# The order of work in the first four chunks of a fused attention and two-MLP kernel

## The chip, the cores and the metric

The kernel runs on one core of a Trainium2 chip. What is measured is the device time of one execution in microseconds. The core has five engines that work side by side, each through its own instructions in their written order: TensorE (PE: matmuls), VectorE (DVE), ScalarE (ACT), GpSimd (POOL) and SyncE (SP), which here only issues loads and stores. They meet through semaphores: an instruction raises one when it is done, and an engine stands still at a wait until the value is there.

## The reference, cut to what matters

```python
# attention, 4 x 8 heads, 576 tokens, head_dim 64, window of 64 tokens
scores = scale * q @ k.T;  scores masked with -1e9 outside the window
attn = exp(scores - rowmax) / (rowsum + 1e-9);  x = attn @ v         # 2304 x 512 tokens
# first MLP ("A"), d_ff 1536
xn = x / sqrt(mean(x * x) + 1e-6) * rms_g
x2 = (silu(xn @ w_gate) * (xn @ w_val)) @ w_out
# second MLP ("B"), d_ff 2048
h = x2 @ w_in;  out = (h * sigmoid(1.702 * h)) @ w_out2
```

All is float32. Each factor is split into a high part (rounded to a type that TensorE takes at full rate) and a low part (the rest), and each product is three matmuls: high by high, low by high, high by low (lines 646 to 649).

## The kernel before, in words

MLP A goes over five tiles of tokens, `TILES_A` (line 38): tile 0 has 256 tokens, the others 512. In each tile it goes over `CA` = 12 chunks of 128 columns of d_ff. A chunk c has three matrices of weights m: gate (0), value (1) and output (2), each 128x512, written here as (c, m). They are loaded in tile 0 only and stay in `w_all`.

**A chunk on TensorE** (lines 747 to 768): `gate(t, c)`, `val(t, c)` of 12 matmuls each, and two chunks later `project_A`, again 12. Between them stands the attention of the next tile, in steps of 256 tokens and two heads: steps 4 to 11 in tile 0 (`EARLY` = 4 steps were done before). A pair of steps is in work over three chunks (`SCORES_AT` = 1, 3, 5, 7): scores after chunk 1, row maxima, exponentials and normalisation with chunk 2, transposes with chunk 3 (line 614), the multiplications by V (`probs_by_v`, line 628), then the next pair's scores (line 600). `probs_by_v(4, 3)` waits until hidden of chunk 2 is made (line 621), since its result goes to the PSUM bank that val of chunk 2 was in. `val(0, 4)` in its turn waits until ScalarE has copied that result away (line 698).

**A chunk on VectorE** in tile 0: `scale_gate` (line 1249), `silu_A` (1254, after ScalarE's tanh), `hidden_A` (1263), `hid_lo_A` (1269, after ScalarE's cast `hid_hi_A`). Between them stand the low halves of the weights two chunks ahead, `weights_lo_A` (line 1218), each of which raises `w_split`, and for a pair of steps `row_max` (1133), `reciprocal_of_sum` (1143, 1145) and `normalise` (1150). `row_max` of a pair waits for the scores of both steps.

**A chunk on ScalarE:** `tanh_A` (line 996), `hid_hi_A` (1006), the high halves of the weights three chunks ahead, `weights_hi_by_act` (920), for a pair of steps `exponentials` (881), `copy_probT` (908) and `evacuate_o` (874). The high halves of the third matrix (m = 2) are GpSimd's (546).

**Loads** are issued by SyncE. The raw weights of chunks c and c + 2 share one staging buffer, so `load_wA(c, m)` (line 402) first waits until (c - 2, m) is split. The wait is for a count, so `FIRST_SPLITS` (line 276) has to hold the order in which VectorE makes its splits. In tile 0, iteration c issues the three loads of chunk c + 3, then q and k of the next pair of steps where there is one, then v.

The orders of the four engines are written out by hand in these loops; there is no planner.

Of the kernel before, what the change touches and what calls it, by code (L numbers as in the profile page):

```python
# [23 lines left out]
def fused_attention_mlps(nc, q_t, k_t, v_win, w_a, rms_g, w_b, out):  # L24
# [5 lines left out]
    CA = w_a.shape[0]  # L30
# [20 lines left out]
    EARLY = 4  # L51
# [15 lines left out]
    with ExitStack() as ctx:  # L67
# [205 lines left out]
        def raw(u, m):  # L273
            return wstage[:, (3 * u + m) * DM:(3 * u + m + 1) * DM]

        FIRST_SPLITS = ((0, 0), (0, 1), (1, 0), (1, 1), (2, 0), (0, 2), (2, 1), (1, 2), (2, 2))

        def splitsA(c, m):
            return FIRST_SPLITS.index((c, m)) + 1 if c < 3 else 3 * c + m + 1

        CASTS_BY_ACT = ((0, 1), (1, 1), (2, 0), (2, 1)) + tuple((c, m) for c in range(3, CA) for m in range(2))
        CASTS_BY_POOL = ((0, 0), (1, 0), (0, 2), (1, 2)) + tuple((c, 2) for c in range(2, CA))
# [108 lines left out]
        @block.sync  # L391
        def _(sp):
            def load_step_qk(s):
                sp.wait_ge(scores_done, s - 1 if s >= EARLY + 2 else s - EARLY + 1)
                load_q(sp, s)
                load_k(sp, s)

            def load_step_v(s):
                sp.wait_ge(pv_done, s - 1 if s >= EARLY + 2 else s - EARLY + 1)
                load_v(sp, s)  # L400

            def load_wA(c, m):
                if c >= 2:
                    sp.wait_ge(w_split, splitsA(c - 2, m))
                sp.dma_start(raw(c % 2, m), w_a[c, :, m * DM:(m + 1) * DM]).then_inc(w_loaded[c % 2][m], 16)

            def load_w2(k):
                g, m = (k // 2 - 1, 1) if k % 2 == 0 and k > 0 else ((k + 1) // 2, 0)
                f = 2 * (g % PB)
                if k >= RAWS:  # L410
                    sp.wait_ge(w2_split, pieces_before(k - RAWS + 1))
                sp.dma_start(raw2(k).rearrange("p (f n) -> p f n", f=2),
                             w_b[f:f + 2, :, m * DM:(m + 1) * DM].rearrange("f p n -> p f n")
                             ).then_inc(w2_loaded[k % RAWS], 16)

            def store_x2(t):
                start, n = TILES_A[t]
                for i in range(2):
                    sp.wait_ge(accA_evacuated[i], 2 * (t + 1))
                sp.dma_start(x2[:, :, start:start + n].rearrange("c p t -> p c t"),  # L420
                             x2stage(t)[:, :, 0:n]).then_inc(x2_stored, 16)

            def load_x2(j):
                wait(sp, xcB_lo, COMBOS * j)
                sp.dma_start(x2raw[:, :, :], x2[:, :, j * TB:(j + 1) * TB].rearrange("c p t -> p c t")
                             ).then_inc(x2_loaded, 16)

            def store_out(j):
                for s in range(SUB):
                    sp.wait_ge(accB_evacuated[s % 2], (SUB // 2) * j + s // 2 + 1)  # L430
                    start = j * TB + s * P
                    sp.dma_start(out[start:start + P, :], yB[:, s, :]).then_inc(out_stored, 16)

            for s in range(EARLY):
                load_q(sp, s)
            sp.dma_start(gcol[:, :], rms_g).then_inc(g_loaded, 16)
            for m in range(3):
                load_wA(0, m)
            for m in range(3):
                load_wA(1, m)  # L440
            load_wA(2, 0)
            for s in (EARLY, EARLY + 1):
                load_step_qk(s)
            load_wA(2, 1)
            for s in (EARLY, EARLY + 1):
                load_step_v(s)
            load_wA(2, 2)

            for t in range(NA - 1):
                for c in range(CA):  # L450
                    if t == 0 and c + 3 < CA:
                        for m in range(3):
                            load_wA(c + 3, m)
                    scored = pair_with_scores_at(t, c - 1)
                    multiplied = pair_with_scores_at(t, c - 3)
                    if scored is not None and scored + 2 < STEPS:
                        load_step_qk(scored + 2)
                        load_step_qk(scored + 3)
                    if multiplied is not None and multiplied + 2 < STEPS:
                        load_step_v(multiplied + 2)  # L460
                        load_step_v(multiplied + 3)
                store_x2(t)

            sp.wait_ge(x2_stored, 16 * (NA - 1))
            load_x2(0)
            for k in range(RAWS):
                load_w2(k)
            load_w2(in_unit(2))
            load_w2(out_unit(1))
            load_x2(1)  # L470
            load_w2(in_unit(3))
            store_x2(NA - 1)
            for g in range(1, NP):
                if g > 1:
                    load_w2(out_unit(g))
                if 1 < g < NP - 2:
                    load_w2(in_unit(g + 2))
                if g == PB:
                    sp.wait_ge(x2_stored, 16 * NA)
                    load_x2(2)  # L480
                if g % PB == 2 and g > PB:
                    store_out(g // PB - 1)
            store_out(NB - 1)
            sp.wait_ge(out_stored, 16 * (TOK // P))
# [383 lines left out]
        def _(act):  # L868
# [139 lines left out]
            def evacuate_A(t):  # L1008
                n = TILES_A[t][1]
                for j in (0, 2):  # L1010
                    act.wait_ge(accA_done, (DC - 1) * t + j + 1)
                    nc.scalar.activation(x2stage(t)[:, j, 0:n], acc_of(t, j), ACT.Copy,
                                         scale=0.5).then_inc(accA_evacuated[0], 1)

            for t in range(NA):
                for c in range(CA):
                    scored = pair_with_scores_at(t, c - 1)
                    transposed = pair_with_scores_at(t, c - 2)
                    multiplied = pair_with_scores_at(t, c - 3)
                    if multiplied is not None:  # L1020
                        evacuate_o(multiplied)
                        evacuate_o(multiplied + 1)
                    if scored is not None:
                        exponentials(scored)
                    if t == 0 and transposed is not None:
                        copy_probT(transposed)
                        copy_probT(transposed + 1)
                    if (t, c) != (0, 1):
                        tanh_A(t, c)
                    if (t, c) == (0, 0):  # L1030
                        tanh_A(0, 1)
                    if c == SUMSQ_AT and t + 1 < NA:
                        sum_hi(t + 1)
                    if scored is not None:
                        exponentials(scored + 1)
                    if t > 0 and transposed is not None:
                        copy_probT(transposed)
                        copy_probT(transposed + 1)
                    hid_hi_A(t, c)
                    if c == SUMSQ_AT and t + 1 < NA:  # L1040
                        inverse_rms(t + 1)
                    if t == 0 and c + 3 < CA:
                        weights_hi_by_act(c + 3, 0)
                        weights_hi_by_act(c + 3, 1)
                    if t == NA - 1 and 4 <= c < 4 + COMBOS:
                        xcB_hi_block(0, c - 4)
                    if t == NA - 1 and c in (7, 9):
                        w2in_hi((c - 7) // 2, range(IN_PIECES))
                    if t == NA - 1 and c == CA - 1:
                        w2out_hi(0, 0)  # L1050
                        w2out_hi(0, 1)
# [66 lines left out]
        def _(dve):  # L1118
# [153 lines left out]
            def evacuate_A(t):  # L1272
                n = TILES_A[t][1]
                for j in range(DC) if t == 0 else (1, 3):
# [8 lines left out]
                    else:  # L1283
                        nc.vector.tensor_scalar(x2stage(t)[:, j, 0:n], acc_of(t, j), 0.5, None,
                                                ALU.mult).then_inc(accA_evacuated[1], 1)

            for t in range(NA):
                for c in range(CA):
                    scored = pair_with_scores_at(t, c - 1)
                    if scored is not None:  # L1290
                        row_max(scored)
                        row_max(scored + 1)
                    split = c + 2 if t == 0 and c + 2 < CA else None
                    if t == 0 and c != 1:
                        scale_gate(c)
                    if t == 0 and c == 0:
                        scale_gate(1)
                        weights_lo_A(2, 1)
                    if scored is not None:
                        reciprocal_of_sum(scored)  # L1300
                        normalise(scored)
                    if split is not None and c > 0 and c != 2:
                        weights_lo_A(split, 0)
                    silu_A(t, c)
                    hidden_A(t, c)
# [7 lines left out]
                    if scored is not None:  # L1313
                        reciprocal_of_sum(scored + 1)
                        normalise(scored + 1)
                    if split is not None and c == 2:
                        weights_lo_A(split, 0)
                    if split is not None and c > 0:
                        weights_lo_A(split, 1)
                    if t == 0 and c == 0:  # L1320
                        weights_lo_A(1, 2)
                    hid_lo_A(t, c)
                    if split is not None:
                        weights_lo_A(split, 2)
# [139 lines left out]
```

## Time and profile before

| | |
|---|---|
| median of 3 runs | 902.53 us (902.11 to 903.44) |
| the profiled execution | 902.16 us, of which the span from the first to the last instruction 900.4 us |
| TensorE busy | 887.5 us (99%), in 5368 matmuls |
| VectorE, ScalarE, GpSimd busy | 540.4, 400.6, 82.2 us |
| TensorE's granted clock | 1.00 (2.4 GHz) in the mean |
| loaded and stored | 69.8 MB |

One execution was recorded by the profiler. The page gives shares over the whole span: by them the kernel is bound by TensorE. The first 90 us (tile 0, in which the weights come in) look different: there the other engines are nearly as busy, and their order of work decides when TensorE gets what it needs. The chain that ended last is 95% TensorE.

### The profile page before, as it was taken

Reading aid. Unit: us, or ns where it says so; the run is one execution under the profiler, and the core shown is the slowest. Engines: PE = TensorE matmul, PEld = TensorE weight load, DVE = VectorE, ACT = ScalarE, POOL = GpSimd, SP = SyncE. Lnnn points to the kernel's source line nnn. Section 1 sums busy time; section 2 is a strip of 40 time slices with the busy share of each in tenths; the row PEclk is TensorE's granted clock in tenths of the full one; section 3 lists DMA queues with packets and bytes.
Section 4 is the critical chain, followed back from the end, with each engine's and each line's share of the span. In section 5 each row is a group of like instructions: output and inputs, shape, how many; then the busy total and the mean of one; then the engine's idle time right before and its main releaser. Section 6 shows DMA issues by size and latency. Waiting matters only on the chain.

```text
span 900.4 us, 14698 instructions
## 1 busy us (share of the span) xinstructions
PE 887.5 (99%) x5368; PEld 769.3 (85%) x5368; DVE 540.4 (60%) x1256; ACT 400.6 (44%) x944; POOL 82.2 (9%) x111
## 2 busy tenths in 40 slices
PE   8899999999999999999999999999999999999998
PEld 7799888888888888888888899999999999999997
DVE  6997533334343344333346578887788788877663
ACT  6766333342333433334123354545464554545442
POOL 5144001030011300112000000000000000000000
PEclk9999999999999999999999999999999999999999
DMA  7672111102111021100400221121432121241201
GB/s 243 214 227 89 51 51 51 50 24 74 51 50 55 20 74 50 51 25 8 179 1 24 94 99 66 68 73 47 164 118 94 48 79 63 70 142 48 70 24 71
DMA packets 41079, 69.77 MB, mean 77 GB/s; under 512 B 3632, under 2 KB 13872, under 8 KB 41008
## 3 DMA queue, kind: packets, MB, share of 16 engines
q1 hardware_dynamic: 39600, 67.12, 23.0%
q10 hardware_dynamic: 1408, 1.70, 0.6%
q8 instruction: 44, 0.72, 0.3%
q14 instruction: 27, 0.22, 0.1%
HBM read 59.38 MB, written 9.44 MB: 76 GB/s over the span
## 4 chain that ended last, share of the span: by engine, by line
PE 95%; ACT 2%; DVE 1%; issue 1%; DMA 0%; POOL 0%; SPq 0%; POOLq 0%; DVEq 0%; ACTq 0%
PE ps L647 16%; PE ps L649 16%; PE ps L648 16%; PE ps L839 7%; PE ps L840 7%; PE ps L838 7%; PE ps L781 7%; PE ps L777 7%; PE ps L779 6%; PE ps L628 2%; PE ps L600 2%; PE ps L614 2%; ACT prob L881 1%; DMA wstage<-in_w_a 0%; ACT xT L881 0%
## 5 line engine op out<-in xcount | busy, mean ns | idle before, releaser
L647 PE MATMUL ps<-x_hi,w_all 128*128 128x512 f32 (+1 forms) x480 | 179.4, 374 | 0.6 <-issue 0.5
L649 PE MATMUL ps<-x_lo,w_all 128*128 128x512 f32 (+1 forms) x480 | 176.7, 368 | 0.0
L648 PE MATMUL ps<-x_hi,w_all 128*128 128x512 f32 (+1 forms) x480 | 176.7, 368 | 0.0
L840 PE MATMUL ps<-w2out,hB 128*128 128x512 f32 x288 | 113.0, 392 | 0.0
L839 PE MATMUL ps<-w2out,hB 128*128 128x512 f32 x288 | 112.9, 392 | 0.0
L838 PE MATMUL ps<-w2out,hB 128*128 128x512 f32 x288 | 112.0, 389 | 0.0
L647 PEld LDWEIGHTS ps<-x_hi,w_all 128*128 128x128 f32 x480 | 90.4, 188 | 19.0 <-issue 3.9
L649 PEld LDWEIGHTS ps<-x_lo,w_all 128*128 128x128 f32 x480 | 90.4, 188 | 15.2
L648 PEld LDWEIGHTS ps<-x_hi,w_all 128*128 128x128 f32 x480 | 90.5, 188 | 14.5
L1254 DVE SCALAR_TENSOR_TENSOR sig<-sig,ps 128x512 f32<-128x512 f32 x48 | 32.9, 686 | 107.1 <-ACT sig L996 107.1
L647 PE MATMUL ps<-h_hi,w_all 128*128 128x512 f32 (+1 forms) x240 | 89.8, 374 | 1.9 <-DVE hid L1263 1.6
L648 PE MATMUL ps<-h_hi,w_all 128*128 128x512 f32 (+1 forms) x240 | 88.4, 368 | 0.0
L649 PE MATMUL ps<-h_lo,w_all 128*128 128x512 f32 (+1 forms) x240 | 88.3, 368 | 0.0
L1263 DVE TENSOR_TENSOR hid<-ps,sig 128x512 f32<-128x512 f32 (+1 forms) x59 | 37.9, 642 | 66.2 <-PE ps L649 52.5
L1006 ACT CAST h_hi<-hid 128x512 fp32r<-128x512 f32 (+1 forms) x60 | 34.8, 580 | 94.1 <-DVE hid L1263 94.1
L781 PE MATMUL ps<-xcB_even,w2in 128*128 128x384 f32 x224 | 75.2, 336 | 0.0
L777 PE MATMUL ps<-xcB_even,w2in 128*128 128x384 f32 x224 | 75.2, 336 | 0.0
L779 PE MATMUL ps<-xcB_even,w2in 128*128 128x384 f32 x224 | 75.0, 335 | 0.0
L996 ACT ACTIVATE sig<-ps 128x512 f32<-128x512 f32 x48 | 28.6, 597 | 103.6 <-PE ps L649 103.4
L840 PEld LDWEIGHTS ps<-w2out,hB 128*128 128x128 f32 x288 | 54.0, 188 | 11.3
L839 PEld LDWEIGHTS ps<-w2out,hB 128*128 128x128 f32 x288 | 54.0, 188 | 10.4
L838 PEld LDWEIGHTS ps<-w2out,hB 128*128 128x128 f32 x288 | 54.1, 188 | 10.2
(148 smaller groups left out, 1555.6 us busy)
## 6 DMA issues: line engine op xcount, KB each, us to landing
wstage<-in_w_b SPq DMA_DIRECT2D x48, 512.0 KB, 3.7
wstage<-in_w_a SPq DMA_DIRECT2D x36, 256.0 KB, 3.5
vwin<-in_v_win SPq DMA_DIRECT2D x32, 256.0 KB, 3.7
kwin<-in_k_t SPq DMA_DIRECT2D x32, 160.0 KB, 3.5
x2raw<-x_scratch SPq DMA_DIRECT2D x3, 1536.0 KB, 6.6
out_dram<-yB SPq DMA_DIRECT2D x18, 256.0 KB, 4.3
qtok<-in_q_t SPq DMA_DIRECT2D x34, 128.0 KB, 2.6
x_scratch<-wstage SPq DMA_DIRECT2D x3, 1024.0 KB, 4.2
```

What stands on the lines that cost most here:

```text
L647: pe.matmul(out_, w[:, 0, cols], xh, start=first, stop=False, **flags)
L648: pe.matmul(out_, w[:, 1, cols], xh, start=False, stop=False, **flags)
L649: return pe.matmul(out_, w[:, 0, cols], xl, start=False, stop=last, **flags)
L777: pe.matmul(out_, w2in[:, g % 2, 0, a_, cols], x[:, b_, 0, d, :], start=fresh and d == 0, stop=False, skip_group_check=True)
L779: pe.matmul(out_, w2in[:, g % 2, 1, a_, cols], x[:, b_, 0, d, :], start=False, stop=False, skip_group_check=True)
L781: ins = pe.matmul(out_, w2in[:, g % 2, 0, a_, cols], x[:, b_, 1, d, :], start=False, stop=last, skip_group_check=True)
L838: pe.matmul(y, h[:, rows], w[:, 0, chunk, :], start=(p == 0 and first), stop=False)
L839: pe.matmul(y, h[:, rows], w[:, 1, chunk, :], start=False, stop=False)
L840: ins = pe.matmul(y, hB_of(g, chunk, 1)[:, rows], w[:, 0, chunk, :], start=False, stop=last)
L1006: nc.scalar.copy(h_hi[:, c % RING, 0:TILES_A[t][1]], hid[:, 0:TILES_A[t][1]]).then_inc(hidA_hi, 1)
L1254: nc.vector.scalar_tensor_tensor(out=silu_of(t, c), in0=silu_of(t, c), scalar=1.0, in1=scaled_of(c) if t == 0 else gate_of(t, c), op0=ALU. ...
L1263: nc.vector.tensor_tensor(hid[:, 0:w], val_of(t, c), silu_of(t, c), ALU.mult).then_inc(hidA_made, 1)
```

## The change

It concerns tile 0, chunks 0 to 3. The loops of VectorE and ScalarE now begin at chunk 4 of tile 0, and what they did before stands written out ahead of them.

- **VectorE:** silu 1 and hidden 1 directly after chunk 0's; row maximum 4, splits (3,0) and (3,1), row maximum 5, reciprocal and normalisation of both steps with split (1,2) between them, then hid_lo 1 and chunk 2. Split (1,2) was made in chunk 0, (2,2) too, (3,2) at the end of chunk 1; they now follow normalise 4, scale_gate 2 and hid_lo 2.
- **ScalarE:** exponentials 4 and 5 back to back (tanh 2 was between them); casts (4,0), (4,1) and both `copy_probT` now come before tanh 2, and casts (5,0), (5,1) before hid_hi 2.
- **SyncE:** the loads of chunk 3 as before. Then (4,0), (4,1), q and k of steps 6 and 7, (5,0), (5,1), (4,2), (5,2), where it was (4,0) to (4,2), (5,0) to (5,2), q and k. From (6,0) on as before.
- `FIRST_SPLITS` holds the new order for six chunks. TensorE and GpSimd keep their orders.

No instruction is added or taken away.

```diff
--- before.py
+++ after.py
@@ -273,10 +273,11 @@
         def raw(u, m):
             return wstage[:, (3 * u + m) * DM:(3 * u + m + 1) * DM]
 
-        FIRST_SPLITS = ((0, 0), (0, 1), (1, 0), (1, 1), (2, 0), (0, 2), (2, 1), (1, 2), (2, 2))
+        FIRST_SPLITS = ((0, 0), (0, 1), (1, 0), (1, 1), (2, 0), (0, 2), (2, 1), (3, 0), (3, 1), (1, 2),
+                        (2, 2), (4, 0), (4, 1), (3, 2), (5, 0), (5, 1), (4, 2), (5, 2))
 
         def splitsA(c, m):
-            return FIRST_SPLITS.index((c, m)) + 1 if c < 3 else 3 * c + m + 1
+            return FIRST_SPLITS.index((c, m)) + 1 if c < 6 else 3 * c + m + 1
 
         CASTS_BY_ACT = ((0, 1), (1, 1), (2, 0), (2, 1)) + tuple((c, m) for c in range(3, CA) for m in range(2))
         CASTS_BY_POOL = ((0, 0), (1, 0), (0, 2), (1, 2)) + tuple((c, 2) for c in range(2, CA))
@@ -448,12 +449,22 @@
 
             for t in range(NA - 1):
                 for c in range(CA):
-                    if t == 0 and c + 3 < CA:
+                    scored = pair_with_scores_at(t, c - 1)
+                    multiplied = pair_with_scores_at(t, c - 3)
+                    if (t, c) == (0, 1):
+                        load_wA(4, 0)
+                        load_wA(4, 1)
+                        load_step_qk(EARLY + 2)
+                        load_step_qk(EARLY + 3)
+                    elif (t, c) == (0, 2):
+                        load_wA(5, 0)
+                        load_wA(5, 1)
+                        load_wA(4, 2)
+                        load_wA(5, 2)
+                    elif t == 0 and c + 3 < CA:
                         for m in range(3):
                             load_wA(c + 3, m)
-                    scored = pair_with_scores_at(t, c - 1)
-                    multiplied = pair_with_scores_at(t, c - 3)
-                    if scored is not None and scored + 2 < STEPS:
+                    if scored is not None and scored + 2 < STEPS and (t, c) != (0, 2):
                         load_step_qk(scored + 2)
                         load_step_qk(scored + 3)
                     if multiplied is not None and multiplied + 2 < STEPS:
@@ -1012,8 +1023,29 @@
                     nc.scalar.activation(x2stage(t)[:, j, 0:n], acc_of(t, j), ACT.Copy,
                                          scale=0.5).then_inc(accA_evacuated[0], 1)
 
+            tanh_A(0, 0)
+            tanh_A(0, 1)
+            hid_hi_A(0, 0)
+            weights_hi_by_act(3, 0)
+            weights_hi_by_act(3, 1)
+            hid_hi_A(0, 1)
+            exponentials(EARLY)
+            exponentials(EARLY + 1)
+            weights_hi_by_act(4, 0)
+            weights_hi_by_act(4, 1)
+            copy_probT(EARLY)
+            copy_probT(EARLY + 1)
+            tanh_A(0, 2)
+            weights_hi_by_act(5, 0)
+            weights_hi_by_act(5, 1)
+            hid_hi_A(0, 2)
+            tanh_A(0, 3)
+            hid_hi_A(0, 3)
+            weights_hi_by_act(6, 0)
+            weights_hi_by_act(6, 1)
+
             for t in range(NA):
-                for c in range(CA):
+                for c in range(4 if t == 0 else 0, CA):
                     scored = pair_with_scores_at(t, c - 1)
                     transposed = pair_with_scores_at(t, c - 2)
                     multiplied = pair_with_scores_at(t, c - 3)
@@ -1025,10 +1057,7 @@
                     if t == 0 and transposed is not None:
                         copy_probT(transposed)
                         copy_probT(transposed + 1)
-                    if (t, c) != (0, 1):
-                        tanh_A(t, c)
-                    if (t, c) == (0, 0):
-                        tanh_A(0, 1)
+                    tanh_A(t, c)
                     if c == SUMSQ_AT and t + 1 < NA:
                         sum_hi(t + 1)
                     if scored is not None:
@@ -1284,22 +1313,54 @@
                         nc.vector.tensor_scalar(x2stage(t)[:, j, 0:n], acc_of(t, j), 0.5, None,
                                                 ALU.mult).then_inc(accA_evacuated[1], 1)
 
+            scale_gate(0)
+            scale_gate(1)
+            weights_lo_A(2, 1)
+            silu_A(0, 0)
+            hidden_A(0, 0)
+            silu_A(0, 1)
+            hid_lo_A(0, 0)
+            hidden_A(0, 1)
+            row_max(EARLY)
+            weights_lo_A(3, 0)
+            weights_lo_A(3, 1)
+            row_max(EARLY + 1)
+            reciprocal_of_sum(EARLY)
+            normalise(EARLY)
+            weights_lo_A(1, 2)
+            reciprocal_of_sum(EARLY + 1)
+            normalise(EARLY + 1)
+            hid_lo_A(0, 1)
+            scale_gate(2)
+            weights_lo_A(2, 2)
+            weights_lo_A(4, 0)
+            silu_A(0, 2)
+            hidden_A(0, 2)
+            weights_lo_A(4, 1)
+            hid_lo_A(0, 2)
+            weights_lo_A(3, 2)
+            scale_gate(3)
+            weights_lo_A(5, 0)
+            silu_A(0, 3)
+            hidden_A(0, 3)
+            weights_lo_A(5, 1)
+            hid_lo_A(0, 3)
+            weights_lo_A(4, 2)
+            weights_lo_A(5, 2)
+
             for t in range(NA):
-                for c in range(CA):
+                for c in range(4 if t == 0 else 0, CA):
                     scored = pair_with_scores_at(t, c - 1)
                     if scored is not None:
                         row_max(scored)
                         row_max(scored + 1)
                     split = c + 2 if t == 0 and c + 2 < CA else None
-                    if t == 0 and c != 1:
+                    if t == 0:
                         scale_gate(c)
-                    if t == 0 and c == 0:
-                        scale_gate(1)
-                        weights_lo_A(2, 1)
                     if scored is not None:
                         reciprocal_of_sum(scored)
                         normalise(scored)
-                    if split is not None and c > 0 and c != 2:
+                    if split is not None:
                         weights_lo_A(split, 0)
                     silu_A(t, c)
                     hidden_A(t, c)
@@ -1313,12 +1374,8 @@
                     if scored is not None:
                         reciprocal_of_sum(scored + 1)
                         normalise(scored + 1)
-                    if split is not None and c == 2:
-                        weights_lo_A(split, 0)
-                    if split is not None and c > 0:
+                    if split is not None:
                         weights_lo_A(split, 1)
-                    if t == 0 and c == 0:
-                        weights_lo_A(1, 2)
                     hid_lo_A(t, c)
                     if split is not None:
                         weights_lo_A(split, 2)
```

## Rows read from the trace of the kernel before

**Rows 1.** waits of TensorE, 0 to 100 us: us in total, times, longest us

```profile
PE ps L614 <- DVE prob L1150: 2.6, 2, 1.6
PE ps L647 <- DVE hid L1263: 1.6, 1, 1.6
...
PE ps L647 <- issue: 0.5, 1, 0.5
```

**Rows 2.** timeline, TensorE: start us, us, engine, line, what [idle before <- what ended it]

```profile
28.93 0.36 PE L647 MATMUL ps<-h_hi,w_all 128*128 128x256 f32 x1 [1.64 <-DVE hid L1263]
...
30.43 0.28 PE L647 MATMUL ps<-x_hi,w_all 128*128 128x256 f32 x1
...
36.68 0.66 PE L614 MATMUL ps<-ident,prob 128*128 128x128 f32 x4 [1.56 <-DVE prob L1150]
...
38.69 1.15 PE L628 MATMUL ps<-probT,vwin 128*64 128x64 f32 x32
...
40.80 0.38 PE L647 MATMUL ps<-x_hi,w_all 128*128 128x256 f32 x1
...
42.62 0.36 PE L647 MATMUL ps<-x_hi,w_all 128*128 128x256 f32 x1
```

**Rows 3.** two stretches: length, busy of PE, PEld, DVE, ACT, POOL, granted clock, DMA share, GB/s

```profile
22.89:41.95 19.06, 14.86 (x188) 13.57 (x187) 17.93 (x51) 12.98 (x36) 3.50 (x4) 1.00 0.69 216
26.00:31.00 5.00, 3.36 (x28) 3.18 (x28) 4.96 (x12) 2.29 (x5) 1.63 (x2) 1.00 0.77 246
```

**Rows 4.** timeline, ScalarE, the same columns

```profile
26.61 1.25 ACT L920 CAST w_all<-wstage 128x512 fp32r<-128x512 f32 x2 [0.73 <-DMA wstage<-in_w_a]
...
31.61 0.40 ACT L881 ACTIVATE prob<-prob,nmax 128x128 f32<-128x128 f32 x1
...
33.17 0.40 ACT L996 ACTIVATE sig<-sig 128x256 f32<-128x256 f32 x1
...
37.00 1.07 ACT L908 COPY probT<-ps 128x512 f32<-128x512 f32 x2
...
41.88 0.64 ACT L874 COPY xT<-ps 128x256 f32<-128x256 f32 x2
```

**Rows 5.** timeline, VectorE

```profile
25.01 0.42 DVE L1263 TENSOR_TENSOR hid<-ps,sig 128x256 f32<-128x256 f32 x1
...
25.95 0.83 DVE L1269 TENSOR_TENSOR h_lo<-hid,h_hi 128x256 fp32r<-128x256 f32 x1
...
35.53 0.16 DVE L1143 TENSOR_SCALAR rrec<-rsum 128x4 f32<-128x4 f32 x1
...
35.93 0.69 DVE L1150 TENSOR_TENSOR prob<-prob,rrec 128x512 f32<-128x512 f32 x1
...
41.01 0.42 DVE L1269 TENSOR_TENSOR h_lo<-hid,h_hi 128x256 fp32r<-128x256 f32 x1
41.35 0.68 DVE L1218 TENSOR_TENSOR w_all<-wstage,w_all 128x512 fp32r<-128x512 f32 x1
...
41.95 0.28 DVE L1133 CUSTOM_DVE_ANT_0 prob<-ps,mask 128x128 f32<-128x128 f32 x1
...
43.64 0.42 DVE L1249 TENSOR_TENSOR sig<-ps,hid 128x256 f32<-128x256 f32 x1
```

**Rows 6.** timeline, SyncE's queue: loads (3,2), (4,0) and (6,0)

```profile
26.06 0.33 SPq L405 DMA_DIRECT2D wstage<-in_w_a  x1
...
26.44 0.43 SPq L405 DMA_DIRECT2D wstage<-in_w_a  x1
...
37.26 0.33 SPq L405 DMA_DIRECT2D wstage<-in_w_a  x1
```

**Rows 7.** chain that ended last, 26 to 28 us: start us, us, what (here (4,1))

```profile
26.91 4.04 DMA wstage<-in_w_a
```

**Rows 8.** loads of weights, 20 to 60 us

```profile
DMA to landing us min/median/max: 2.6/3.4/5.2
```

**Rows 9.** timeline, GpSimd

```profile
25.39 1.12 POOL L546 CAST w_all<-wstage 128x512 fp32r<-128x512 f32 x1 [3.35 <-DMA wstage<-in_w_a]
```

## The prediction

> **What bounds the kernel now.** I read first who TensorE waited for in the first 100 us [rows 1], then TensorE in order of time [rows 2]. TensorE is busy 99% of the span, so only its idle time can be won. In the stretch that the change touches it is idle three times: 1.64 us before the first projection (it waits for hidden 1 on VectorE), and 2.6 us in two waits for the normalised probabilities of steps 4 and 5, the second ending at 36.68. That is 4.2 us and the most the change can give. From 22.89 to 41.95, from the first scaled gate to the last split of chunk 5, VectorE is busy 17.93 of 19.06 us [rows 3]: it is the engine whose order decides. Later, val of chunk 4 starts at 42.62, right after ScalarE's two copies of the attention output, which end at 42.52 [rows 2, 4].
>
> **The lengths of the steps.** A row's length overlaps the next start; I use the distance between starts. VectorE: low half of a split (L1218) 0.60, 256-column operation 0.34, two row maxima 1.69, reciprocal 0.40, normalise 0.61 [rows 5]. ScalarE: exponentials of a step 1.56, a cast or a copy of 512 columns 0.52, one of 256 columns 0.32 [rows 4]. TensorE: 12 matmuls of 256 columns 1.5 at most (28.93 to 30.43), a transpose of a step's four blocks 0.41 (36.68 to project 1), multiplications by V and scores 2.1 together (38.69 to 40.80) [rows 2]. A load is issued 0.38 to 0.47 after the one before it [rows 6, 7] and lands 2.6, 3.4 or 5.2 us later (least, median, most) [rows 8]; the third of a burst took 4.04 [rows 7].
>
> **Part 1, VectorE's order up to the transposes: the gain.** Hidden 0 starts at 25.01 as before. Next comes silu 1 (25.36), whose tanh is ready, then hid_lo 0, which waits for ScalarE's cast until 25.9 and may again take 0.83 beside a GpSimd cast, as it does now [rows 5, 9]; hidden 1 then ends at 26.8 to 27.2 where it now ends just before 28.93 [rows 2]. Project 0 can start at 27.3, not 28.93: 1.6 us won. Row maximum 4 ends at 28.0; casts (3,0), (3,1) end at 27.9 as before [rows 4]; exponentials 4 run 28.1 to 29.8, splits (3,0), (3,1) and row maximum 5 until 30.0, exponentials 5 from 30.1 to 31.8. Normalise 4 ends at 31.1, split (1,2) at 31.7, normalise 5 at 32.9. TensorE, through gate 3 and val 3 at 31.7, transposes step 4 at once and step 5 at 32.9 instead of 36.68: 3.75 us ahead, project 1 done near 34.9. If nothing came later, that would be the result.
>
> **Part 2, the queue of loads: what I think undoes it.** Loads wait on SyncE, in order. Load (3,2) waits for split (1,2), since both use one staging buffer. Now split (1,2) comes early, and load (3,2) leaves at 26.06, with (4,0) right behind at 26.44 although its own buffer was free long before [rows 6]. In the new order split (1,2) is the tenth, behind normalise 4, and ends at 31.7. So (3,2) leaves at 31.7, (4,0) at 32.1, (4,1) at 32.6: 5.7 us later than now. With the landings of now (the burst of 26.06 shifted by 5.7 us) (4,1) lands at 36.2 to 36.6.
>
> **Part 3, ScalarE's casts and copies in front of tanh 2.** ScalarE now does casts (4,0), (4,1), both probT copies, then tanh 2. Cast (4,1) waits for the landing at 36.2 to 36.6 and takes 0.5, the copies 1.05, tanh 0.4: tanh 2 ends at 38.2 to 38.7. Queued behind: silu 2 and hidden 2 on VectorE, 0.9 us, so 39.1 to 39.6. The multiplications by V of step 4 write the bank that val 2 leaves, so they wait for hidden 2: TensorE, ready at 34.9, stands 4.3 us and starts them at 39.1 to 39.6, against 38.69 now. The whole gain of part 1 is spent, and 0.4 to 0.9 more. Scores 6, 7 and gate 4 then take the time they take now, and val 4 could start at 42.7 to 43.2.
>
> **Part 4, the same again for chunk 6.** Behind (4,1) SyncE issues four loads of q and k (0.58 MB) and then (5,0), (5,1) at 34.9 and 35.4, which land between 38.0 (least) and 40.6 (most); the 1.9 MB from (3,2) on at the 246 GB/s of the present burst [rows 3] take 7.7 us from 31.7, which speaks for 39.5, and I take that. ScalarE has casts (5,0), (5,1) ahead of hid_hi 2: hid_hi 2 ends near 40.5, hid_lo 2 near 40.9, split (3,2) near 41.5. Load (5,2) waits for this split, and (6,0), (6,1) stand behind it: they leave at 41.9 and 42.3, against 37.26 now for the first [rows 6]. (6,1) lands 3.4 to 4.0 later, at 45.7 to 46.3; its cast (0.5) and the two evacuations of step 4 and 5 (0.64) come ahead of val 4, which starts at 46.9 to 47.6, against 42.62: 4.3 to 5.0 us late. TensorE stands a second time for about 4 us. VectorE's last split, (5,2), ends near 45.5 against 41.95, so its later work moves along.
>
> **What follows.** After val 4 the pattern of two chunks repeats, set by TensorE; of waits that could take up a delay I find only 0.46 us before val 6 (the "issue" wait of rows 1, again behind the copies of the attention output). So 4.3 to 5.0 less up to 0.5: +4.4. The profiled span 900.4 becomes 904.8, its execution 902.16 becomes 906.6, and with the median of 902.53 (0.37 above the profiled one) **907.0 us**. Bounds: with every load landing after 2.6 us the same chain gives tanh 2 at 36.9, split (3,2) at 39.7, (6,1) at 43.2, val 4 at 44.4: +1.8 (904.3). With 5.2 each: tanh 2 at 39.8, split (3,2) at 42.7, (6,1) at 48.7, val 4 at 50.0: +7.4 (909.9). I take the middle because the third of a burst and not the lone load is what is waited for. The parts that are neither removed nor added (number of instructions, bytes) cost nothing: the work is the same.
>
> **Rivals.**
> (a) *Faster: the loads come in time.* If (4,1) landed by 33.5 and (6,1) by 40, the gain of 3.75 us would stay; with the slack before val 4 and 6 and a little lost on VectorE, which has 1.1 us idle in 19 [rows 3], -3.6: 898.9 us. For it: the splits are put in TensorE's order, and (5,0) to (5,2) have their loads in the order of the splits. Against it: (3,2) is not moved behind (4,0), (4,1). It decides whether SyncE issues (4,0) before 29. Chance 0.12.
> (b) *No change: the delay is met halfway.* Landings near the least and VectorE making up what ScalarE loses: within 1.8 us, 902.5. It needs split (3,2) by 38. Chance 0.08.
> (c) *Slower, as forecast:* 907.0, chance 0.65, with 904.3 to 909.9.
> (d) *Slower still, by TensorE's clock.* The granted clock is 1.00 over the whole stretch [rows 3] and the longest wait in this stage 1.64 us [rows 1, 2]; the change makes two stands of about 4 us each. If the clock fell to 1.2 GHz after one of them, each group of 12 matmuls would take up to 1.5 us more; after the first stand this is hidden by the wait for val 4, after the second two groups would cost 3.0: 910.0 us, up to 912 with a third. The Trainium skill, TensorE: Matmul & The Clock Gate, Part 1, says that activity releases a throttle which idleness brings back; by it this case would come about, and nothing in this trace can confirm it, since no row shows a lower clock. Chance 0.15.
> (e) *That the change doesn't do what it says* is contained in (a) to (c): the order is written out, but "loads in an order to match" holds for chunk 5 only.
>
> **How the numbers follow.** Measured to about 0.2% (1.8 us) either way. Slower: (c) and (d), 0.80. Same: (b), 0.08. Faster: (a), 0.12. The range leaves out (a), the half of (b) below no change (0.04) and the far end of (d), and takes in the rest: 902.5 to 911.0.
>
> **What would show it.** Part 1: project 0 near 27.3 and the second transpose near 33. Part 2: SyncE idle between (3,1) and (3,2) until split (1,2) ends near 31.7. Part 3: TensorE idle before the multiplications by V of step 4, tanh 2 after ScalarE's wait for (4,1). Part 4: ScalarE waiting for (6,0), (6,1) and val 4 near 47. It is wrong if (4,0) leaves before 29, if those multiplications start before 37, or if a later stage of tile 0 gives back over 1 us.

## The result, and the profile after

| | before | after |
|---|---|---|
| median, 6 runs each | 902.93 us (902.11 to 903.50) | 908.79 us (907.22 to 910.01) |
| the profiled execution | 902.16 us, span 900.4 | 907.86 us, span 905.8 |
| TensorE busy | 887.5 us | 889.0 us |
| VectorE, ScalarE, GpSimd busy | 540.4, 400.6, 82.2 us | 540.4, 400.6, 81.6 us |

The ratio is 1.0068, 95% interval 1.0057 to 1.0078: the changed kernel is slower by 5.9 us in the median and by 5.4 us of span in the profiled executions. The other engines do the same work. The span less TensorE's busy time is 12.9 us before the change and 16.8 after it; in the other 1.5 us TensorE is busy for longer, 1.3 of them by its clock, below. The time of an execution is 1.8 to 3.1 us more than its span, in the kernel before as in the others, so medians that differ by less than 1 us are compared by their spans too.

In the changed kernel the lines after the loops of SyncE have moved on by 11 (L647 is L658, L628 is L639) and VectorE's by 29 (L1218 is L1247). Who TensorE waited for in the first 100 us (us in total, times, longest), to be read beside [rows 1]:

```profile
PE ps L639 <- DVE hid L1292: 4.9, 1, 4.9
PE ps L658 <- issue: 3.1, 2, 3.0
...
PE ps L625 <- DVE prob L1179: 1.0, 2, 0.6
```

The wait for hidden 1 is gone and the one for the normalised probabilities is 1.0 instead of 2.6 us. In their place stand one wait of 4.9 us and one of 3.0 us; I call such a wait a stand. TensorE in order of time, against [rows 2]:

```profile
27.31 0.36 PE L658 MATMUL ps<-h_hi,w_all 128*128 128x256 f32 x1
...
32.93 0.66 PE L625 MATMUL ps<-ident,prob 128*128 128x128 f32 x4 [0.62 <-DVE prob L1179]
33.36 0.36 PE L658 MATMUL ps<-h_hi,w_all 128*128 128x256 f32 x1
...
39.96 1.97 PE L639 MATMUL ps<-probT,vwin 128*64 128x64 f32 x32 [4.94 <-DVE hid L1292]
...
43.33 0.38 PE L658 MATMUL ps<-x_hi,w_all 128*128 128x256 f32 x1
...
47.98 0.35 PE L658 MATMUL ps<-x_hi,w_all 128*128 128x256 f32 x1 [2.96 <-issue]
```

Project 0 starts at 27.31 (28.93 before), the transpose of step 5 at 32.93 (36.68), the multiplications by V of step 4 at 39.96 (38.69), val 4 at 47.98 (42.62). A lead of 3.75 us at 33 has become a lag of 5.36 us at 48. The page called "issue" what it cannot name; the chain of waits of the same stretch names it (start us, us, what):

```profile
31.03 0.69 DVE w_all L1247
...
31.74 0.33 SPq L406
...
32.11 0.43 SPq L406
...
32.59 0.43 SPq L406
...
33.06 0.43 SPq L379
...
34.48 0.43 SPq L383
...
34.96 4.34 DMA wstage<-in_w_a
...
39.32 0.62 ACT w_all L931
...
40.48 0.41 ACT h_hi L1017
...
40.91 0.04 DVE h_lo L1298
...
41.42 0.68 DVE w_all L1247
...
42.97 3.72 DMA wstage<-in_w_a
...
46.72 0.04 ACT w_all L931
...
47.24 0.24 ACT xT L885
```

To be read downwards: split (1,2) ends at 31.72 and releases load (3,2); SyncE issues (4,0), (4,1), four loads of q and k, then (5,0), which takes 4.34 us; its cast; hid_hi 2 (L1017) behind the cast; hid_lo 2 (L1298); split (3,2) at 41.42; behind load (5,2) and (6,0), load (6,1), 3.72 us; its cast at 46.72; the two evacuations from 47.24; and then val 4. Of what [rows 6] shows, (6,0) left at 37.26 before.

TensorE's clock is what the windows show (length, busy of PE, PEld, DVE, ACT, POOL, granted clock, DMA share, GB/s):

```profile
34.00:39.00 5.00, 1.02 (x9) 0.82 (x7) 0.84 (x2) 2.52 (x5) 0.61 (x1) 1.00 1.00 337
40.00:42.00 2.00, 2.00 (x36) 1.88 (x40) 1.60 (x3) 0.88 (x2) 0.61 (x1) 0.50 0.01 4
44.00:47.00 3.00, 1.02 (x9) 0.81 (x7) 2.49 (x9) 1.17 (x3) 1.02 (x1) 1.00 0.72 223
48.00:60.00 12.00, 12.00 (x144) 11.43 (x144) 10.93 (x29) 8.11 (x28) 5.92 (x9) 1.00 0.70 233
```

After the stand from 35.0 to 39.96 the granted clock is 0.50 (1.2 GHz), where [rows 3] had 1.00 throughout. The 32 matmuls by V took 1.97 us instead of 1.15, and gate 4 begins 3.37 us after their start instead of 2.11. It costs nothing there, since val 4 is not ready until 47.98. After the second stand of 2.96 us it is 1.00 in this execution.

### The profile page after: what moved, and what is told of

It reads as the page before. It is cut to its first block, busy times and chain, and to the rows that moved or that the text cites. A ratio compares the mean times of both kernels' runs of the same rounds, so it can differ in the third digit from the quotient of the medians.

```text
span 905.8 us, 14698 instructions
## 1 busy us (share of the span) xinstructions
PE 889.0 (98%) x5368; PEld 771.2 (85%) x5368; DVE 540.4 (60%) x1256; ACT 400.6 (44%) x944; POOL 81.6 (9%) x111
## 4 chain that ended last, share of the span: by engine, by line
PE 93%; DVE 3%; ACT 2%; issue 1%; DMA 1%; SPq 0%; ACTq 0%; DVEq 0%
PE ps L658 16%; PE ps L660 15%; PE ps L659 15%; PE ps L850 7%; PE ps L851 7%; PE ps L849 7%; PE ps L792 6%; PE ps L788 6%; PE ps L790 6%; PE ps L639 2%; PE ps L611 2%; PE ps L625 1%; DMA wstage<-in_w_a 1%; DVE w_all L1247 1%; ACT prob L892 1%
## 5 line engine op out<-in xcount | busy, mean ns | idle before, releaser
L658 PE MATMUL ps<-x_hi,w_all 128*128 128x512 f32 (+1 forms) x480 | 179.4, 374 | 3.2 <-issue 3.1
L658 PEld LDWEIGHTS ps<-x_hi,w_all 128*128 128x128 f32 x480 | 90.3, 188 | 21.6 <-issue 6.5
L1283 DVE SCALAR_TENSOR_TENSOR sig<-sig,ps 128x512 f32<-128x512 f32 x48 | 32.9, 686 | 107.1 <-ACT sig L1007 107.1
L658 PE MATMUL ps<-h_hi,w_all 128*128 128x512 f32 (+1 forms) x240 | 89.8, 374 | 0.2 <-DVE h_lo L1298 0.2
L1017 ACT CAST h_hi<-hid 128x512 fp32r<-128x512 f32 (+1 forms) x60 | 34.8, 580 | 93.1 <-DVE hid L1292 93.1
```

Source lines behind the costliest of these rows:

```text
L658: pe.matmul(out_, w[:, 0, cols], xh, start=first, stop=False, **flags)
L1017: nc.scalar.copy(h_hi[:, c % RING, 0:TILES_A[t][1]], hid[:, 0:TILES_A[t][1]]).then_inc(hidA_hi, 1)
L1283: nc.vector.scalar_tensor_tensor(out=silu_of(t, c), in0=silu_of(t, c), scalar=1.0, in1=scaled_of(c) if t == 0 else gate_of(t, c), op0=ALU. ...
```

## The experiments

Each time is the median of its runs, and each ratio is against the kernel before on the same chip in the same job (902.58, 902.55 and 902.64 us in the three jobs). I name two theories throughout. L: the wait of load (3,2) on SyncE, and the loads queued behind it, are the cause. A: ScalarE's new order alone is.

### One load moved

```diff
 (0, 0): load_wA(3, 0); load_wA(3, 1)
-        load_wA(3, 2)
 (0, 1): load_wA(4, 0); load_wA(4, 1)
+        load_wA(3, 2)
         load_step_qk(6); load_step_qk(7)
```

> The changed kernel with one load moved: (3,2) goes behind (4,0) and (4,1), ahead of q and k of steps 6 and 7. Theory L (the wait of load (3,2) on SyncE holds (4,0), (4,1) and through them everything): (4,0) leaves near 24 instead of 32.1, tanh 2 ends near 34.5, the multiplications by V of step 4 start near 35.6 instead of 39.96. But q and k now wait behind (3,2) and land near 37, and (5,0), (5,1) near 38, so val 4 starts near 45.6 instead of 47.98: about 2.5 us faster than the changed kernel, 905 to 907, still slower than before. Rival A (ScalarE's order alone, casts ahead of tanh, is what costs): no more than 1 us less than the changed kernel, over 907.5. Rival C (TensorE's clock is the larger part): the first stand shrinks, the granted clock stays at 1.00, and the time falls to 903 to 904 even though val 4 still waits.

Measured: 908.9 us, ratio 1.0066 (1.0051 to 1.0081). As slow as the changed kernel: my range for L was missed by 2 us, and the number by itself is the one that I had given to A. The trace shows why it doesn't speak for A. TensorE, and the cast of (5,0) and (5,1) on ScalarE:

```profile
36.55 1.15 PE L643 MATMUL ps<-probT,vwin 128*64 128x64 f32 x32 [0.58 <-DVE hid L1296]
...
38.97 0.67 PE L615 MATMUL ps<-kwin,qtok 64*64 64x128 f32 x16 [0.66 <-DMA kwin<-in_k_t]
...
48.07 0.55 PE L662 MATMUL ps<-x_hi,w_all 128*128 128x256 f32 x1 [6.82 <-issue]
```

```profile
39.62 1.24 ACT L935 CAST w_all<-wstage 128x512 fp32r<-128x512 f32 x2 [4.14 <-DMA wstage<-in_w_a]
```

The first stand is gone (0.58 us instead of 4.94; the multiplications by V start 3.4 us earlier), and val 4 has not moved (48.07 and 47.98), nor has the end. So the first stand, which I had taken for the place where the gain is spent, is not on the chain that sets the end. The second is, now 6.82 us long: (5,0) and (5,1) still stand behind (3,2), are cast at 39.62 and hold hid_hi 2. The scores of step 7 wait 0.66 us for k besides, because q and k now stand behind (3,2). Another difference is small: here the clock fell in the second stand (0.50 in 46 to 50) and project 3 starts at 56.08 instead of 54.60, but the span is only 0.3 us longer (906.1 and 905.8).

### The two stands apart

On top of the last kernel, hid_hi 2 goes ahead of casts (5,0), (5,1) on ScalarE:

```diff
 tanh_A(0, 2)
+hid_hi_A(0, 2)
 weights_hi_by_act(5, 0)
 weights_hi_by_act(5, 1)
-hid_hi_A(0, 2)
```

> As e1_three_two_behind (load (3,2) behind (4,0) and (4,1)), and hid_hi 2 ahead of casts (5,0) and (5,1) on ScalarE. That run had the first stand almost gone and was as slow as the changed kernel. Theory L2 (what decides is the chain (5,1) landing, cast, hid_hi 2, hid_lo 2, split (3,2), load (6,1), cast, evacuation, val 4, and the first stand costs nothing by itself): split (3,2) ends near 37.9 instead of 42.4, (6,1) leaves near 38.7, val 4 starts near 43.8: 903.5 to 904.5. If the second stand has another cause: above 907.

Measured: 905.84 us, ratio 1.0035 (1.0021 to 1.0048). Two thirds of what I expected: taking the chain away moved val 4 from 48.07 to 44.59, but I had put it at 43.8 and the time at 903.5 to 904.5. The 0.8 us have a cause of their own. Casts (6,0) and (6,1) no longer wait for their loads:

```profile
39.80 1.29 ACT L935 CAST w_all<-wstage 128x512 fp32r<-128x512 f32 x2 [3.01 <-DMA wstage<-in_w_a]
...
42.81 1.13 ACT L935 CAST w_all<-wstage 128x512 fp32r<-128x512 f32 x2
```

The first row is (5,0) and (5,1), which land late as before and now hold tanh 3 (40.99) and with it hidden 3, hid_hi 3 (42.50) and the casts of the second row. The clock fell too. Two of TensorE's matmuls after the stand of 3.12 us, and a window:

```profile
47.56 0.41 PE L662 MATMUL ps<-h_hi,w_all 128*128 128x256 f32 x1
47.77 0.41 PE L663 MATMUL ps<-h_hi,w_all 128*128 128x256 f32 x1
```

```profile
46.00:50.00 4.00, 4.00 (x24) 4.00 (x23) 3.36 (x12) 3.09 (x16) 2.81 (x6) 0.59 0.93 325
```

They start 0.21 us apart, where 128x256 matmuls stand 0.12 apart elsewhere, and the granted clock of 46 to 50 is 0.59. To price that I filled the stand:

```diff
 def val(t, c):
+    if (t, c) == (0, 4):
+        pe.wait_ge(gate_scaled, 4)
+        keep_busy(0, 12)        # ps[:, 0, 0:128] <- ones, ones
```

> As e9_hid_hi_first, with 12 matmuls whose results nobody reads ahead of val 4 (they fill the second stand and add nothing to the result). In e9_hid_hi_first val 4 started 2.0 us later than before the change, but project 3 started 3.2 us later: in between some 16 matmuls came 0.21 apart instead of 0.12. Theory K (that difference is TensorE's clock, which fell after the stand of 3.1 us): the granted clock is 1.00 after the stand, the matmuls after val 4 are 0.12 apart, project 3 starts near 51.4 instead of 52.69, and the time is 904.3 to 904.8 against 905.8. If the slow matmuls have another cause (loads landing, weights not ready): 905.5 or more.

Measured: 904.74 us, ratio 1.0023 (1.0014 to 1.0032). The window of 46 to 50 now shows

```profile
46.00:50.00 4.00, 4.00 (x36) 4.00 (x35) 3.36 (x11) 2.98 (x16) 2.71 (x6) 1.00 0.99 312
```

36 matmuls instead of 24, at clock 1.00. Val 4 starts at 44.46 instead of 44.59 and project 3 at 52.05 instead of 52.69 (51.4 expected). So theory K is right about the slow matmuls. Their price is not the 1.1 us between the two medians. The median spans are 902.9 and 903.1 us, both profiled executions have a span of 903.0, and the intervals of the two ratios overlap; 0.9 of the 1.1 us lie outside the span. Further on in the same stage, first the kernel before the filling, then the filled one:

```profile
84.61 0.50 PE L657 MATMUL ps<-ss_hi,ones_r 128*128 128x512 f32 x1 [0.79 <-DVE ss_lo L1376]
```

```profile
84.59 0.50 PE L657 MATMUL ps<-ss_hi,ones_r 128*128 128x512 f32 x1 [0.91 <-DVE ss_lo L1379]
```

The lead is gone: the filled kernel waited 0.72 us for the probabilities of step 7 and 0.45 before val 6, the other had neither wait. By the median spans the fall of the clock cost 0.2 us, which is within their scatter.

### The same filling in the changed kernel

19 such matmuls ahead of the multiplications by V of step 4 (into bank 4), 16 ahead of val 4 (into bank 1, after hidden 3).

> The changed kernel with matmuls whose results nobody reads in its two stands: 19 ahead of the multiplications by V of step 4 and 16 ahead of val 4. They fill the waiting time and add nothing to the result. Theory L with a small part for the clock: the granted clock stays at 1.00 in every window, the stands end when they ended, val 4 still starts near 48, and the time is 907.5 to 908.3, that is the 5.4 us of the profiled run of the changed kernel and not the 5.9 of its median; the scatter of the runs shrinks. Rival C (the clock is a large part): 905 or less. If the matmuls get in the way: over 909.

Measured: 907.92 us, ratio 1.0062 (1.0049 to 1.0074); the runs span 907.49 to 908.98, those of the changed kernel 907.22 to 910.01. Against its own before it is 5.4 us slower, the changed kernel 5.9. The granted clock is 1.00 in every window from 26 to 62, and val 4 starts at 48.26. So the clock is at most about half a microsecond of the loss (0.35 by the median spans, 906.1 against 906.45), and the intervals of the two ratios overlap, so even that is not shown. The mechanism of the rest is not the clock.

### The split, not the load, moved

```diff
-FIRST_SPLITS = (..., (2, 1), (3, 0), (3, 1), (1, 2), ...)
+FIRST_SPLITS = (..., (2, 1), (1, 2), (3, 0), (3, 1), ...)
 hidden_A(0, 1)
+weights_lo_A(1, 2)
 row_max(4)
...
 normalise(4)
-weights_lo_A(1, 2)
```

> The changed kernel with the order of the loads left alone and split (1,2) put back early on VectorE, between hidden 1 and row maximum 4 (its place in the list of splits is moved with it). Theory L: it is the wait of load (3,2) that matters, not its place; (3,2) leaves near 27.7, (4,0) near 28.1, val 4 starts near 43.2, against 47.98 and 42.62 before the change: 0 to 1 us slower than before (903 to 904.5). The transposes of step 5 come 0.6 us later than in the changed kernel (33.5). Rival A: within 1 us of the changed kernel, above 907.5.

Measured: 903.94 us, ratio 1.0015 (1.0005 to 1.0024). The order of the loads and ScalarE's order are those of the changed kernel; 0.6 us of VectorE's work stands elsewhere, and three quarters of the loss are gone. Load (3,2) from the chain of waits, then TensorE:

```profile
27.69 0.33 SPq L406
```

```profile
36.10 1.15 PE L639 MATMUL ps<-probT,vwin 128*64 128x64 f32 x32 [0.57 <-DVE hid L1292]
...
43.51 0.36 PE L658 MATMUL ps<-x_hi,w_all 128*128 128x256 f32 x1 [3.60 <-issue]
```

This is the run that settles L: what matters is the count that load (3,2) waits for. Of the 1.4 us that remain, 0.9 are in the same chain: (6,1) is cast at 42.24, and val 4 is 0.9 us later than before the change. The clock fell after this stand too (0.70 in 46 to 50); its share was not separated.

### ScalarE's order alone

```diff
 exponentials(4); exponentials(5)
-weights_hi_by_act(4, 0); weights_hi_by_act(4, 1)
 copy_probT(4); copy_probT(5)
 tanh_A(0, 2)
+weights_hi_by_act(4, 0)
+hid_hi_A(0, 2)
+weights_hi_by_act(4, 1)
 weights_hi_by_act(5, 0); weights_hi_by_act(5, 1)
-hid_hi_A(0, 2)
```

> The changed kernel with its own order of loads, but ScalarE's order turned back in chunk 2: after the exponentials both probT copies, tanh 2, cast (4,0), hid_hi 2, casts (4,1), (5,0), (5,1). Theory L: (4,0) and (4,1) still leave SyncE at 32.1 and 32.6; tanh 2 ends near 34.5, split (4,0) is ready at 36.6, hidden 2 ends near 37.5 and the multiplications by V start at 37.5 instead of 39.96, but split (3,2) comes near 40.1 and (6,1) leaves near 40.9, so val 4 starts near 45.9: 905 to 906, between before and the changed kernel. Rival A (ScalarE's order alone costs the 5.9 us): 902.6 to 903.5. Rival C (the clock): as 903 to 904, since the first stand is below 3 us.

Measured: 905.68 us, ratio 1.0037 (1.0023 to 1.0050), and the multiplications by V start at 37.27, val 4 at 45.49. ScalarE's order is worth about half of the loss while the loads are late; it cannot mend it, because (6,1) still leaves behind split (3,2). Theory A as the whole cause is out (it said 902.6 to 903.5). This half and the three quarters of the last run overlap: late loads hurt through the casts that stand ahead of tanh 2 and hid_hi 2, and with every load in time the same order of casts costs nothing measurable (ratio 1.0000, below).

### Loads in time, and what is next

The loads of chunks 4 and 5 and the q and k of steps 6 and 7 ahead of (3,2):

```diff
-3,0  3,1  3,2  4,0  4,1  q6 k6 q7 k7  5,0  5,1  4,2  5,2  6,0 ...
+3,0  3,1  4,0  4,1  q6 k6 q7 k7  5,0  5,1  3,2  4,2  5,2  6,0 ...
```

> The changed kernel with the loads in the order (3,0), (3,1), (4,0), (4,1), q and k of steps 6 and 7, (5,0), (5,1), (3,2), (4,2), (5,2), then (6,0) on as before. Theory L: nothing waits for chunks 4 and 5 any more; hidden 2 ends near 35.5, split (3,2) near 37.1, but (6,0), (6,1) still stand behind (5,2) and leave at 37.5 and 37.9, as in the kernel before the change, so val 4 starts at 42.2 to 42.9 and the time is that of before within 1 us (902 to 904). My rival (a) of the prediction said -3.6 for loads in time (899.3); theory L says it was too bold, because (6,1) and VectorE's own amount of work are next. Rival A: 906 or more.

Measured: 903.68 us, ratio 1.0011 (1.0001 to 1.0021); val 4 at 43.74, 0.8 us later than expected, after a stand of 3.40 us and with the clock at 0.81 and 0.76 in the two windows from 42 to 50. Then (6,0), (6,1) ahead of (5,2) as well:

> As e2_loads_in_time, and (6,0), (6,1) ahead of (5,2), (6,2) behind it. Theory L: val 4 no longer waits for (6,1); what is next is VectorE, whose last split of this stage, (5,2), ends near 41.2 against 41.95 before: 0.7 to 1.6 us faster than before (901.3 to 902.3). If VectorE were not the next bound, as rival (a) of the prediction had it, 899.3.

Measured: 902.78 us, ratio 1.0000 (0.9991 to 1.0010): the time of before, 0.5 us over the range that I gave. TensorE:

```profile
42.36 0.36 PE L666 MATMUL ps<-x_hi,w_all 128*128 128x256 f32 x1 [1.60 <-issue]
...
49.61 0.66 PE L633 MATMUL ps<-ident,prob 128*128 128x128 f32 x4 [0.82 <-DVE prob L1187]
```

Val 4 starts at 42.36, still after a wait of 1.6 us (its two evacuations stand behind casts (6,0), (6,1)), and the transpose of step 7 waits 0.82 us for VectorE. The longest stand is 1.60 us and the clock stays at 1.00. So with every load in time the order of the change gains nothing measurable.

Theory D said that VectorE's work ahead of the normalisation of steps 6 and 7 is next. Two moves on top:

```diff
 hid_lo_A(0, 3)
-weights_lo_A(4, 2); weights_lo_A(5, 2)
 row_max(6); row_max(7)
+weights_lo_A(4, 2); weights_lo_A(5, 2)
...
 hid_hi_A(0, 3)
+evacuate_o(4); evacuate_o(5)
 weights_hi_by_act(6, 0); weights_hi_by_act(6, 1)
-evacuate_o(4); evacuate_o(5)
```

> As e6_six_ahead, and VectorE makes row maxima 6 and 7 ahead of splits (4,2) and (5,2), and ScalarE evacuates steps 4 and 5 ahead of casts (6,0) and (6,1). Theory D (with the loads in time VectorE's amount of work up to the normalisation of steps 6 and 7 sets the end, and the rest of the gain of part 1 is lost there): val 4 starts without a wait near 40.6, normalise 7 ends 1.3 us earlier than in e6_six_ahead, so project 3 starts near 48.7 against 50.0 there and 49.45 before: 901.5 to 902.3, 0.3 to 1 us faster than before. If something after it is next: as before, 902.6.

Measured: 903.3 us, ratio 1.0009 (1.0000 to 1.0017), above the 901.5 to 902.3 of theory D and also above the 902.6 of its rival, and no gain on the last kernel. The middle of it came true (project 3 starts at 47.39 instead of 50.02, and 49.45 before the change), the end did not:

```profile
50.17 0.69 PE L647 MATMUL ps<-probT,vwin 128*64 128x64 f32 x16 [1.10 <-issue]
51.46 0.77 PE L647 MATMUL ps<-probT,vwin 128*64 128x64 f32 x16 [0.61 <-DMA vwin<-in_v_win]
52.16 1.99 PE L619 MATMUL ps<-kwin,qtok 64*64 64x128 f32 x32
```

The multiplications by V of step 6 begin after 1.10 us, those of step 7 after 0.61 us more for v. The scores behind them took 1.99 us for 1.10: the clock had fallen here too. The loads of v stood behind (6,2), (7,0), (7,1), (7,2), two of which wait for the splits that I had just moved back. One more order of loads:

```diff
 load_wA(6, 0); load_wA(6, 1); load_wA(5, 2)
+load_step_v(6); load_step_v(7)
 load_wA(6, 2)
 load_wA(7, 0); load_wA(7, 1); load_wA(7, 2)
 load_step_qk(8); load_step_qk(9)
-load_step_v(6); load_step_v(7)
```

> As e7_vector_relieved, with the loads of v for steps 6 and 7 ahead of (6,2) instead of behind (7,2). In e7_vector_relieved project 3 started 2.1 us earlier than before the change, and all of it was lost again before the multiplications by V of steps 6 and 7 (waits of 1.10 and 0.61 us, the second for v). Theory D2 (that loss is the queue on SyncE once more): those multiplications start near 49.0 and 49.5, without the loss, and the time is 901.0 to 902.0, 0.5 to 1.5 us faster than before. If the lead is given back once more further on (the casts of the next weights, whose loads are as late as before): within 0.5 us of 902.6.

Measured: 901.03 us, ratio 0.9983 (0.9974 to 0.9992): 1.6 us faster than before the change (1.4 by the median spans, 899.1 against 900.5), and the whole interval lies below 1.

```profile
48.13 0.36 PE L668 MATMUL ps<-h_hi,w_all 128*128 128x256 f32 x1
...
49.73 1.15 PE L649 MATMUL ps<-probT,vwin 128*64 128x64 f32 x32
```

Project 3 and the multiplications by V follow each other without a wait. This is the fastest kernel of the study. That the lead of 2.1 us at project 3 in the kernel before it was lost to the loads of v and to the clock together was shown only as a sum; the two were not separated.

## Why the prediction was right, and where it was not

**What bounds.** Right. What TensorE could win was its idle time, and the most that was won is 1.6 of the 4.2 us, with further moves on VectorE, on ScalarE and in the queue of loads.

**Part 1, the gain.** Right to 0.1 us: project 0 at 27.31 (27.3 predicted), the second transpose at 32.93 (32.9), split (1,2) done at 31.7 (31.7).

**Part 2, the queue.** Right: (3,2) left at 31.74, (4,0) at 32.11, (4,1) at 32.59 (31.7, 32.1, 32.6). The run with the split moved shows that this wait is the cause of most of the loss.

**Part 3, the casts ahead of tanh 2.** Right in mechanism, 0.3 to 0.5 us short in size, wrong in weight. Here are ScalarE's casts (4,0) and (4,1), tanh 2 and the next casts:

```profile
35.31 0.62 ACT L931 CAST w_all<-wstage 128x512 fp32r<-128x512 f32 x1 [3.57 <-DMA wstage<-in_w_a]
37.09 0.62 ACT L931 CAST w_all<-wstage 128x512 fp32r<-128x512 f32 x1 [1.16 <-DMA wstage<-in_w_a]
...
38.56 0.43 ACT L1007 ACTIVATE sig<-sig 128x256 f32<-128x256 f32 x1
39.32 1.25 ACT L931 CAST w_all<-wstage 128x512 fp32r<-128x512 f32 x2 [0.33 <-DMA wstage<-in_w_a]
```

(4,1) was cast at 37.09, 4.5 us after it left (36.2 to 36.6 predicted), tanh 2 ended at 38.99 (38.2 to 38.7), the multiplications by V started at 39.96 (39.1 to 39.6). But I wrote that the whole gain of part 1 is spent there. The run with one load moved took this stand away and the time stayed. Two paths lead to hid_hi 2, by (4,1) and hidden 2, and by (5,0), (5,1) and their casts; they arrived within a microsecond of each other (39.9 and 40.5), and the second decides even alone. I had both in the text and did not ask what would remain if one went. The forecast did not suffer from it, since its sum starts from the second path, the landing of (5,0) and (5,1).

**Part 4, the chain to val 4.** Right in each link, and short in two terms. Both casts (5,0) and (5,1) stood behind a landing at 39.30, so hid_hi 2 ended at 40.88 instead of 40.5; hid_lo 2 took 0.51 from start to start beside a GpSimd cast, not 0.34. So split (3,2) ended at 42.10 instead of 41.5 and (6,1) left at 42.97 instead of 42.3; it landed after 3.72 us, inside the 3.4 to 4.0. Val 4 started at 47.98 against 46.9 to 47.6.

**What follows: the terms that were mis-sized.** The forecast was the middle of part 4, 4.65 us, less 0.25 for the wait before val 6. Val 4 was 5.36 us late, 0.7 more. The wait before val 6 did shrink (0.46 to 0.18 us), but a new one of 0.38 us for the probabilities of step 9 took its place, so nothing came off. That makes the 5.4 us of longer span. The median moved by 5.9; the last half microsecond is the clock or the time outside the span, and no run separates them. In absolute numbers 907.0 was forecast and 908.79 measured: 1.4 us of this are the change, 0.4 are the kernel before, whose median was 902.93 here and 902.53 there.

**The rivals.** (a), faster: what was to decide it, (4,0) out before 29, was false in the changed kernel and was made true in eight of the ten experiments (28.06 with the split moved, earlier than that in the others). Its price of -3.6 us was wrong. The two that bring all loads of chunks 4 and 5 in time came out at 1.0011 and 1.0000, because (6,1) and then VectorE were next; I had given VectorE's 1.1 us of idle time as nearly no obstacle to a lead of 3.75 us. (b) did not happen. (d), the clock: it fell after a stand of 4.9 us, where it was hidden as predicted. (The Trainium skill, TensorE: Matmul & The Clock Gate, Part 1, by which idleness brings the throttle back, agrees with that row.) After the second stand it did not fall in the profiled execution. In the kernel where it fell after a stand ahead of val 4 and was priced, some 16 matmuls stood 0.21 apart instead of 0.12, one group and a third and not two; that is 1.4 us, and later waits took up all but 0.2 of it. The price of 3.0 was wrong by both.

## What to carry to other kernels

When steps are reordered on one engine, follow every semaphore count that they raise to the queue that waits for it. A load that reuses a buffer is tied to the last reader of that buffer, and all loads behind it on the same queue are tied with it, so the order of the loads has to follow the new order of the splits, not the chunk numbers. A stand that is seen is not yet a stand that costs: take it away and look at the end, because a second path may arrive at the same time. And where two medians differ by a microsecond, look whether their spans differ too.

## What was not expected of the hardware

In the profiled executions the granted clock fell with the first stand of the changed kernel (4.94 us) and with the stands ahead of val 4 of 6.82, 3.86, 3.60, 3.40 and 3.12 us in five experiments (one load moved, ScalarE's order alone, the split moved, loads in time, hid_hi 2 first). It did not fall after the changed kernel's 2.96 us. In four of the five the matmuls still stood 0.12 apart for 0.7 to 1.5 us after the stand and only then 0.21. It was 1.00 throughout this stretch of the kernel before, whose longest wait here was 1.64 us. In the kernel with VectorE relieved it fell although no single wait was longer than 1.10 us:

```profile
46.00:50.00 4.00, 2.91 (x24) 2.47 (x22) 3.97 (x8) 2.85 (x6) 3.33 (x6) 1.00 0.99 342
50.00:54.00 4.00, 3.22 (x64) 2.75 (x64) 2.98 (x5) 2.19 (x5) 2.60 (x4) 0.74 0.95 337
```

There TensorE was busy for 2.91 and 3.22 of 4 us in two windows on end. In the kernel before it was busy for less, in one such window, and the clock stayed:

```profile
34.00:38.00 4.00, 1.98 (x15) 1.74 (x16) 3.90 (x9) 3.46 (x11) 0.64 (x1) 1.00 0.27 88
```

What exactly makes it fall is not settled by these runs. Filling the waits with matmuls that nobody reads kept the clock at 1.00 in both kernels in which it was tried, and shortened the median span by 0.2 and 0.35 us, which is within the scatter of the runs. A fall of the clock is easily seen in a window and costs little where later waits take it up.
